# Moving a gate chain from GpSimd to VectorE, ahead of the first probabilities, with DMA reordering behind it

## Chip, cores and metric

One Trainium2 chip, one core. The metric is the device time of one execution in microseconds (us). The kernel before was timed three times: 417.96, 418.92 and 419.44 us, median 418.92. TensorE is called PE in the rows, VectorE DVE, ScalarE ACT, GpSimd POOL, and SyncE SP; "q" behind an engine's name is its instruction queue.

## The reference, cut to what matters

```python
# attention part: B=2 batches, H=8 heads, S=768 steps, D=40
for t in range(S):
    m_new  = max(f_gate[:, :, t] + m, i_gate[:, :, t])
    f_stab = exp(f_gate[:, :, t] + m - m_new)
    i_stab = exp(i_gate[:, :, t] - m_new)
    m = m_new
    C = f_stab * C + i_stab * outer(v_t, k_t)
    n = f_stab * n + i_stab * k_t
    y[:, :, t] = sigmoid(o_gate[:, :, t]) * (C @ q_t) / maximum(abs(n @ q_t), 1.0)
# mixture part: x = y as 1536 tokens x 320, E=4 experts, F=1024
p = domain_probs / (domain_probs.sum(-1) + 1e-9)
out = sum(p[:, e:e+1] * (maximum(x @ w1[e], 0) @ w2[e]) for e in range(4))
```

## The kernel before

**Tiling.** The sequence is cut into 6 chunks of 128 steps. A unit k is one chunk of one batch with its 8 heads, so there are 12 units; units 0 and 1 are the first chunks of the two batches and have nothing to carry in, units 2 to 11 are the "later units". Within a unit the recurrence is written as masked attention: scores q·k on TensorE (`first_scores`, `scores`), a decay factor per pair of steps made on ScalarE (`decays`), masked to the causal half on GpSimd (`causal`, L415), multiplied on VectorE (`probs`, L739), and taken against v on TensorE (`outputs`, L1030). `gate_x` (L757 to L769, VectorE) divides and applies the output gate, `transpose_x` (L1049 to L1051, TensorE), `xt_high` (ScalarE) and `xt_low` (VectorE) turn the result into the mixture's input.

**Gates.** The decays need, for each of 16 rows (batch, head) of the first chunks and for each of 80 rows (chunk, batch, head) of the later ones, a running maximum m and running sums. The first chunks' gate work is at the very start of VectorE's program. For the later ones, `local_maxima` scans within each chunk, `move_ends` (TensorE) brings the chunk ends to 16 rows, `unit_starts` (VectorE) scans over chunks, `move_starts` (TensorE) brings the results back to 80 rows, and `unit_maxima` (VectorE, L723 to L728) finishes m. Then GpSimd does `unit_steps` (L475 to L478), VectorE `gate_scan(1)` (L660, L665), and GpSimd `unit_sums` (L485, L486). The sums are stored to a tensor in DRAM (`g_dram`) and loaded back from it spread over 128 partitions (`load_g`, L296) or over the rows of the carried state (`load_carry`, L304), since `decays` of unit k needs them in that form. The gates' tiles are cut out of the tensor y_acc while it is free, so their rows read `y_acc`.

**Mixture.** The experts' weights come in pairs of slices (`load_pair`, 704 KB each, into `w_raw`, four pairs held at a time). Each slice w is split into a rounded high part on ScalarE (`split_high`, w_hi, L573) and a remainder (w_lo), whose 384 up columns are made on GpSimd (`split_low`, L441) and whose 320 down columns on VectorE (`split_down_low`, L776) for the first 20 slices. 128 slots M follow: in each, TensorE does `up` of a slot ahead (L1074, 8 products: high·high, low·high, high·low), ScalarE `relu`, VectorE `hidden_low` (L808), and TensorE `down(M)` (L1093). Slice w = M + 4 is split in slot M for M below 12. The work of units 2 to 11 is hung on slots: unit 2 has its first decays in slot 1, its second in slot 2, its outputs in slot 5.

**What sets the order.** Every engine's order is written out by hand, with semaphore waits; nothing is scheduled by a program. The orders around the change, before:

```python
# SP, L330-L344                              # VectorE, L831-L839
load_q(2)                                    probs(0, 0); probs(0, 1)
wait(gate_tiles[1]["ready"], 2)              unit_maxima()
store g_dram, 3 DMAs                         probs(1, 0); probs(1, 1)
load_q(3)                                    copy_keys(0, 0, U0, acc_ps[2])
wait(gate_tiles[1]["stored"], 48)            gate_x(0)
load_g(2)                                    gate_scan(1)
...                                          gate_x(1)
```

`keep_clock(n)` on TensorE multiplies a tile of ones by itself and stores nothing that is used. A tensor `*_ps` is a bank of PSUM. `d_exp` counts finished `decays`, `d_masked` finished `causal`, `p_ready` finished `probs`, `out_done` finished `outputs`.

Of the kernel before, what the change touches and what calls it, by code (L numbers as in the profile page):

```python
# [16 lines left out]
U0, U1 = B * H, NU - B * H  # L17
# [114 lines left out]
def build(nc, qk_f, qk_a, qk_s, q_p, kv_n, o_n, fi_rows, fi_units, dom_p, w_b, out):  # L132
# [4 lines left out]
    with ExitStack() as ctx:  # L137
# [143 lines left out]
        def _(sp):  # L281
# [55 lines left out]
            load_q(3)  # L337
            sp.wait_ge(gate_tiles[1]["stored"], 3 * 16)
            load_g(2)
            sp.wait_ge(out_done, 1)  # L340
            sp.wait_ge(add_done, 1)
            load_kv(sp, 2)
            load_carry(2)
            load_pair(sp, 3)  # L344
# [39 lines left out]
        def _(pool):  # L384
# [84 lines left out]
            def unit_steps():  # L469


                gt = gate_tiles[1]
                pool.wait_ge(m_ready, 1)
                pool.wait_ge(local_ready, 3)
                nc.gpsimd.tensor_tensor(gt["fm"][:, :], gt["w"][:, :], m_u[:, :], ALU.add).then_inc(unit_step, 1)  # L475
                pool.wait_ge(unit_step, 1)
                nc.gpsimd.tensor_scalar(gt["g"][:, :], gt["fm"][:, :], 0.0, None, ALU.min).then_inc(unit_step, 1)
                nc.gpsimd.tensor_scalar(gt["j"][:, :], gt["fm"][:, :], 0.0, -1.0, ALU.max, ALU.mult).then_inc(unit_step, 1)  # L478

            def unit_sums():  # L480

                gt = gate_tiles[1]
                pool.wait_ge(gt["step"], 2)
                pool.wait_ge(unit_step, 3)
                nc.gpsimd.tensor_tensor(gt["w"][:, :], gt["j"][:, :], gt["gg"][:, 0, :], ALU.subtract).then_inc(gt["ready"], 1)  # L485
                nc.gpsimd.tensor_scalar(gt["gg"][:, 1, :], gt["gg"][:, 0, :], gt["g"][:, 0:1], None, ALU.add).then_inc(gt["ready"], 1)  # L486

# [8 lines left out]
            unit_steps()  # L496
            weigh_keys(0)
            weigh_keys(1)
            unit_sums()
# [19 lines left out]
        def _(act):  # L519
# [79 lines left out]
            act.dma_start(dp[:, :, :], dom_p).then_inc(dp_in, 16)  # L599
            xt_high(0)  # L600
            xt_high(1)
            split_high(2, None)
            split_high(3, None)
# [27 lines left out]
        def _(dve):  # L631
# [98 lines left out]

            local_maxima()
            unit_starts()

# [99 lines left out]
            unit_maxima()  # L833
            probs(1, 0)
            probs(1, 1)
            copy_keys(0, 0, U0, acc_ps[2])
            gate_x(0)
            gate_scan(1)
# [73 lines left out]
        def _(pe):  # L912
# [100 lines left out]
            def outputs(k):  # L1013
# [7 lines left out]
                elif k == 1:  # L1021
                    pe.wait_ge(gate_tiles[0]["key_tok"], 1)
                elif k == B:
                    pe.wait_ge(decay_step, 3)
                else:
                    pe.wait_ge(xt_done, k)
# [79 lines left out]
            exponents_first(0, 1)  # L1106
            exponents_first(1, 0)
            exponents_first(1, 1)
            move_ends()
# [93 lines left out]
```

## Time and profile before

| | us |
|---|---|
| median of 3 runs | 418.92 |
| the profiled execution's own time | 419.46 |
| its span | 417.6 |
| TensorE busy in the span | 412.4 |
| VectorE, ScalarE, GpSimd busy | 180.2, 158.7, 152.3 |
| granted TensorE clock, mean | 0.999 |

The span begins with the first instruction recorded and ends with the last; 1.86 us of the execution's time lie around it. Busy time is the sum over instructions with overlaps counted once; a matmul's end is modelled, so that a busy TensorE may still hold small waits that show as a longer instruction.

### The profile page before, as it was taken

What the parts mean: (1) busy time and instruction counts of PE and PEld (TensorE: products, weight loads), DVE (VectorE), ACT (ScalarE), POOL (GpSimd) and SP (SyncE); (2) the same over time, 40 slices, a digit from 0 to 9 for tenths busy, and PEclk for the clock granted to TensorE, in tenths of its full rate; (3) what the DMA queues carried; (4) which work ended last, traced back from release to release, by engine and by line L of the source; (5) the groups of instructions that cost most, each with busy time, mean ns of one, the idle gap of its engine ahead of it and who ended that gap; (6) DMA issues with size and microseconds to landing.
All of it is one profiled execution on the core that took longest, in us unless ns stands there. A gap on an engine that the chain in (4) does not pass through costs nothing.

```text
span 417.6 us, 7049 instructions
## 1 busy us (share of the span) xinstructions
PE 412.4 (99%) x2710; PEld 398.7 (95%) x2710; DVE 180.2 (43%) x371; ACT 158.7 (38%) x329; POOL 152.3 (36%) x189
## 2 busy tenths in 40 slices
PE   8999999999999999999999999999999999999997
PEld 8889999999999999999999999999999999999996
DVE  5875786746554656446233231323113122131142
ACT  4575468745354644414112431143211333111111
POOL 4855835494175935304010660065100444000000
PEclk9999999999999999999999999999999999999999
DMA  7889929677513835400000232023200000010010
GB/s 268 271 261 378 390 86 346 248 267 273 187 55 104 311 129 206 129 2 1 2 2 0 75 133 71 0 71 139 71 0 2 0 0 2 0 65 0 2 63 33
DMA packets 16899, 48.45 MB, mean 116 GB/s; under 512 B 1921, under 2 KB 8594, under 8 KB 15714
## 3 DMA queue, kind: packets, MB, share of 16 engines
q1 hardware_dynamic: 16290, 46.60, 31.7%
q10 hardware_dynamic: 576, 1.40, 1.0%
q8 instruction: 22, 0.36, 0.4%
q14 instruction: 11, 0.09, 0.1%
HBM read 45.94 MB, written 2.05 MB: 115 GB/s over the span
## 4 chain that ended last, share of the span: by engine, by line
PE 94%; DMA 2%; DVE 1%; ACT 1%; POOL 1%; issue 1%; SPq 0%; DVEq 0%; POOLq 0%
PE hid_ps L1074 40%; PE acc_ps L1093 36%; PE out_ps L1030 5%; PE score_ps L1093 3%; PE out_ps L1037 2%; PE score_ps L974 2%; PE hid_ps L923 1%; PE add_ps L1009 1%; PE acc_ps L1074 1%; DMA g_all<-g_dram 1%; DMA g_dram<-y_acc 1%; PE score_ps L969 1%; ACT dec_w L552 0%; PE out_ps L1049 0%; PE out_ps L1051 0%
## 5 line engine op out<-in xcount | busy, mean ns | idle before, releaser
L808 DVE SCALAR_TENSOR_TENSOR h_lo<-hid_ps,h_hi 128x384 fp32r<-128x384 f32 (+2 forms) x120 | 68.0, 566 | 220.2 <-ACT h_hi L587 220.0
L587 ACT ACTIVATE h_hi<-hid_ps 128x384 fp32r<-128x384 f32 (+2 forms) x120 | 59.8, 498 | 233.6 <-PE hid_ps L1074 233.5
L1093 PE MATMUL acc_ps<-w_hi,h_hi 128*128 128x320 f32 x352 | 110.4, 314 | 0.1
L1093 PE MATMUL acc_ps<-w_hi,h_lo 128*128 128x320 f32 x352 | 108.8, 309 | 0.0
L1093 PE MATMUL acc_ps<-w_lo,h_hi 128*128 128x320 f32 x352 | 108.3, 308 | 0.0
L1074 PE MATMUL hid_ps<-xt_hi,w_lo 128*128 128x384 f32 (+2 forms) x360 | 103.8, 342 | 0.6 <-POOL w_lo L441 0.6
L1074 PE MATMUL hid_ps<-xt_hi,w_hi 128*128 128x384 f32 (+2 forms) x360 | 104.2, 344 | 0.1
L441 POOL TENSOR_TENSOR w_lo<-w_raw,w_hi 128x384 fp32r<-128x384 f32 x56 | 58.8, 1052 | 118.5 <-ACT w_hi L573 118.5
L1074 PEld LDWEIGHTS hid_ps<-xt_hi,w_lo 128*128 128x128 f32 x360 | 65.4, 189 | 4.9 <-POOL w_lo L441 0.8
L1093 PEld LDWEIGHTS acc_ps<-w_hi,h_hi 128*128 128x128 f32 x352 | 66.3, 188 | 1.6 <-DVE h_lo L808 0.3
L1093 PEld LDWEIGHTS acc_ps<-w_lo,h_hi 128*128 128x128 f32 x352 | 66.3, 188 | 1.3
L1093 PEld LDWEIGHTS acc_ps<-w_hi,h_lo 128*128 128x128 f32 x352 | 66.0, 188 | 0.0
L1074 PEld LDWEIGHTS hid_ps<-xt_hi,w_hi 128*128 128x128 f32 x360 | 62.4, 188 | 1.8 <-ACT w_hi L573 0.2
L1074 PE MATMUL hid_ps<-xt_lo,w_hi 128*128 128x384 f32 (+2 forms) x240 | 62.6, 342 | 0.0
L573 ACT ACTIVATE w_hi<-w_raw 128x704 fp32r<-128x704 f32 x56 | 43.6, 783 | 5.1 <-DMA w_raw<-in_w_b 5.1
L1074 PEld LDWEIGHTS hid_ps<-xt_lo,w_hi 128*128 128x128 f32 x240 | 42.7, 188 | 2.9 <-DVE xt_hi L800 0.2
L415 POOL TENSOR_SCALAR_AFFINE_SELECT dec_w<-dec_w 128x512 f32<-128x512 f32 x22 | 15.1, 685 | 60.1 <-ACT dec_w L552 60.1
L446 POOL TENSOR_TENSOR w_lo<-w_raw,w_hi 128x320 fp32r<-128x320 f32 x36 | 32.5, 902 | 0.0
L552 ACT ACTIVATE dec_w<-g_all,w_tok 128x128 f32<-128x128 f32 x80 | 25.4, 390 | 0.5 <-DMA g_all<-g_dram 0.5
L749 DVE TENSOR_TENSOR split_qk<-raw,split_qk 40x1024 fp32r<-40x1024 f32 x16 | 22.1, 1381 | 0.2
L1030 PE MATMUL out_ps<-kv,prob 128*128 128x41 f32 (+2 forms) x176 | 21.1, 280 | 0.1
L1030 PEld LDWEIGHTS out_ps<-kv,prob 128*128 128x128 f32 x176 | 20.5, 192 | 0.3 <-DVE prob L739 0.3
(171 smaller groups left out, 372.2 us busy)
## 6 DMA issues: line engine op xcount, KB each, us to landing
w_raw<-in_w_b SPq DMA_DIRECT2D x27, 704.0 KB, 4.1
raw<-in_qk_s SPq DMA_DIRECT2D x8, 1024.0 KB
g_all<-g_dram SPq DMA_DIRECT2D x10, 512.0 KB, 6.0
kv<-in_kv_n SPq DMA_DIRECT2D x12, 352.0 KB, 5.4
q_pack<-in_q_p SPq DMA_DIRECT2D x10, 192.0 KB, 6.1
out_y<-y_acc SPq DMA_DIRECT2D x12, 160.0 KB, 1.8
carry<-g_dram SPq DMA_DIRECT2D x30, 60.0 KB
y_acc<-in_o_n SPq DMA_DIRECT2D x1, 1280.0 KB, 12.3
```

Source lines behind the costliest of these rows:

```text
L415: nc.gpsimd.affine_select(out=d, in_=d, compare_op=ALU.is_ge, fill=0.0, base=0, pattern=[[0, HALF], [1, L]], channel_multiplier=-1).then_i ...
L441: up_low = nc.gpsimd.tensor_tensor(w_lo[:, f, 0:384], w_raw[:, at, 0:384], w_hi[:, f, 0:384].bitcast(fp32), ALU.subtract)
L446: nc.gpsimd.tensor_tensor(w_lo[:, f, 384:WB], w_raw[:, at, 384:WB], w_hi[:, f, 384:WB].bitcast(fp32), ALU.subtract).then_inc(w_lo_done, 1)
L552: last = nc.scalar.activation(dec(k, half)[:, a, :], e, ACT.Exp, bias=w_tok[:, k * H + h:k * H + h + 1])
L573: nc.scalar.activation(w_hi[:, f, :], w_raw[:, at, :], ACT.Copy).then_inc(w_hi_done, 1)
L587: nc.scalar.activation(h_hi[:, M % RING, 0:cols], hid_bank(M)[:, 0:cols], ACT.Relu).then_inc(hid_hi, 1)
L749: nc.vector.tensor_tensor(hi, raw[rows, kept(k), t, :, :], hi.bitcast(fp32), ALU.subtract)\
L808: nc.vector.scalar_tensor_tensor(h_lo[:, M % RING, 0:cols], hid_bank(M)[:, 0:cols], 0.0, h_hi[:, M % RING, 0:cols].bitcast(fp32), ALU.max, ...
L974: last = nc.tensor.matmul(bank[:, a * L:(a + 1) * L], split_qk[:, kept(k), 1, h, :], split_qk[:, kept(k), 0, h, :], start=True, stop=True)
L1030: last = nc.tensor.matmul(bank[:, h * DA:(h + n) * DA], prob[:, kept(k), half, at, :], values(k, h, n), start=(k < B or h == 0), stop=True ...
L1074: last = nc.tensor.matmul(hid_bank(M)[:, 0:tiles * L], w, x, start=(i == 0), stop=(i == len(terms) - 1))
L1093: last = nc.tensor.matmul(acc_ps[t][:, 0:DM], x, w, start=(f == 0 and i == 0), stop=(f == NF - 1 and i == 2))
```

## The change

- VectorE now does all gate work of the later units. `unit_maxima` and `unit_steps` come ahead of `probs(0, 0)`, `gate_scan(1)` between the probabilities of unit 0 and those of unit 1, `unit_sums` behind those of unit 1. GpSimd's program loses these five instructions.
- TensorE does `move_ends` two groups of exponents sooner and `move_starts` ahead of both `first_scores`.
- The keys' weights of the first units are turned into `hid_ps[0]` instead of `acc_ps[2]`. So `outputs(1)`, which writes `acc_ps[2]`, waits for `w_tok` only, and `keep_clock(2)` waits for `key_tok`.
- ScalarE splits slices 2 and 3 ahead of `xt_high(0)` and `xt_high(1)` instead of behind them.
- SP issues pair 3 of the weights right behind the gates' store, and `load_carry(2)` right behind `load_g(2)`.

```diff
@@ SP
-            load_q(3)
+            load_pair(sp, 3)
             sp.wait_ge(gate_tiles[1]["stored"], 3 * 16)
             load_g(2)
+            load_carry(2)
+            load_q(3)
             sp.wait_ge(out_done, 1)
             sp.wait_ge(add_done, 1)
             load_kv(sp, 2)
-            load_carry(2)
-            load_pair(sp, 3)
             load_g(3)
@@ GpSimd (the two functions are moved to VectorE, nc.gpsimd becomes nc.vector)
-            def unit_steps():
...
-            def unit_sums():
...
             causal(1, 1)
-            unit_steps()
             weigh_keys(0)
             weigh_keys(1)
-            unit_sums()
@@ ScalarE
+            split_high(2, None)
+            split_high(3, None)
             xt_high(0)
             xt_high(1)
-            split_high(2, None)
-            split_high(3, None)
@@ VectorE
+            def unit_steps():
+                gt = gate_tiles[1]
+                dve.wait_ge(m_ready, 1)
+                dve.wait_ge(local_ready, 3)
+                nc.vector.tensor_tensor(gt["fm"][:, :], gt["w"][:, :], m_u[:, :], ALU.add).then_inc(unit_step, 1)
+                dve.wait_ge(unit_step, 1)
+                nc.vector.tensor_scalar(gt["g"][:, :], gt["fm"][:, :], 0.0, None, ALU.min).then_inc(unit_step, 1)
+                nc.vector.tensor_scalar(gt["j"][:, :], gt["fm"][:, :], 0.0, -1.0, ALU.max, ALU.mult).then_inc(unit_step, 1)
+
+            def unit_sums():
+                gt = gate_tiles[1]
+                dve.wait_ge(gt["step"], 2)
+                nc.vector.tensor_tensor(gt["w"][:, :], gt["j"][:, :], gt["gg"][:, 0, :], ALU.subtract).then_inc(gt["ready"], 1)
+                nc.vector.tensor_scalar(gt["gg"][:, 1, :], gt["gg"][:, 0, :], gt["g"][:, 0:1], None, ALU.add).then_inc(gt["ready"], 1)
             local_maxima()
             unit_starts()
+            unit_maxima()
+            unit_steps()
...
             probs(0, 0)
             probs(0, 1)
-            unit_maxima()
+            gate_scan(1)
             probs(1, 0)
             probs(1, 1)
-            copy_keys(0, 0, U0, acc_ps[2])
+            unit_sums()
+            copy_keys(0, 0, U0, hid_ps[0])
             gate_x(0)
-            gate_scan(1)
             gate_x(1)
@@ TensorE, in outputs(k)
                 elif k == 1:
-                    pe.wait_ge(gate_tiles[0]["key_tok"], 1)
+                    pe.wait_ge(gate_tiles[0]["w_tok"], 1)
@@ TensorE
             exponents_first(0, 1)
+            move_ends()
             exponents_first(1, 0)
             exponents_first(1, 1)
-            move_ends()
+            move_starts()
             first_scores(0)
-            move_starts()
             first_scores(1)
             outputs(0)
             pe.wait_ge(g0["exp"], 1)
             pe.wait_ge(g0["w_tok"], 1)
-            turn(g0, "key", acc_ps[2], U0, U0, "key_ps")
+            pe.wait_ge(m_begun, 1)
+            turn(g0, "key", hid_ps[0], U0, U0, "key_ps")
             outputs(1)
             transpose_x(0)
             additions(0)
+            pe.wait_ge(g0["key_tok"], 1)
             keep_clock(2)
```

The order of VectorE's instructions from `unit_starts` to the start of `gate_x(1)`, before (line numbers of the kernel before; L739 is `probs`, L723 to L728 `unit_maxima`, L689 `copy_keys`, L757 to L769 `gate_x(0)`, L660 and L665 `gate_scan(1)`):

```order
L714 COPY y_acc<-hid_ps0 16x4
L716 SCALAR_TENSOR_TENSOR y_acc<-y_acc,hid_ps0 16x4
L739 TENSOR_TENSOR prob<-score_ps,dec_w 128x512
L739 TENSOR_TENSOR prob<-hid_ps1,dec_w 128x512
L723 TENSOR_TENSOR y_acc<-hid_ps0,y_acc 80x5
L725 TENSOR_REDUCE y_acc<-y_acc 80x1
L728 SCALAR_TENSOR_TENSOR y_acc<-y_acc 80x127
L739 TENSOR_TENSOR prob<-acc_ps0,g_all 128x512
L739 TENSOR_TENSOR prob<-acc_ps1,g_all 128x512
L689 COPY key_w<-acc_ps2 128x16
L757 TENSOR_SCALAR floor<-out_ps 128x8
```

The same stretch of VectorE in the changed kernel (its own line numbers: L702 to L707 `unit_maxima`, L716 to L719 `unit_steps`, L738 `probs`, L644 `gate_scan(1)`, L725 and L726 `unit_sums`):

```order
L702 TENSOR_TENSOR y_acc<-hid_ps0,y_acc 80x5
L704 TENSOR_REDUCE y_acc<-y_acc 80x1
L707 SCALAR_TENSOR_TENSOR y_acc<-y_acc 80x127
L716 TENSOR_TENSOR y_acc<-y_acc 80x128
L718 TENSOR_SCALAR y_acc<-y_acc 80x128
L719 TENSOR_SCALAR y_acc<-y_acc 80x128
L738 TENSOR_TENSOR prob<-score_ps,dec_w 128x512
L738 TENSOR_TENSOR prob<-hid_ps1,dec_w 128x512
L644 SCALAR_TENSOR_TENSOR y_acc<-ones,y_acc 80x127
L738 TENSOR_TENSOR prob<-acc_ps0,g_all 128x512
L725 TENSOR_TENSOR y_acc<-y_acc 80x128
L726 TENSOR_SCALAR y_acc<-y_acc 80x128
```

Six instructions of 80 rows now stand ahead of the first probabilities, a scan between the two units' probabilities, and two more ahead of the copy of the keys' weights (`copy_keys`, which follows).

SP's queue behind the gates' store (L335, L336), the difference of the two orders:

```order
 L335 DMA g_dram<-y_acc 80x128 x2
 L336 DMA g_dram<-y_acc 1x128
+L278 DMA w_raw<-in_w_b 128x1408
+L296 DMA g_all<-g_dram 128x1024
+L304 DMA carry<-g_dram 40x3x128 x3
 L310 DMA q_pack<-in_q_p 128x384
-L296 DMA g_all<-g_dram 128x1024
 L269 DMA kv<-in_kv_n 128x704
-L304 DMA carry<-g_dram 40x3x128 x3
-L278 DMA w_raw<-in_w_b 128x1408
 L296 DMA g_all<-g_dram 128x1024
```

Pair 3 moves past three loads and the wait for the store; the three loads of the carry move past one load of keys and values.

## Rows read from the trace of the kernel before

**Rows 1.** TensorE's waits in the whole span: us in total, times, longest.
```profile
PE hid_ps L1074 <- POOL w_lo L441: 0.6, 1, 0.6
PE acc_ps L1030 <- DVE key_w L689: 0.4, 1, 0.4
```

**Rows 2.** Chain that ended last, pieces: start us, us, what.
```profile
9.48 0.30 PE score_ps L987
...
11.99 1.98 PE out_ps L1030 x16
...
16.92 0.60 POOL y_acc L486
...
30.37 1.01 POOL w_lo L441
```

**Rows 3.** TensorE's timeline: start us, us, what, [idle before <- releaser].
```profile
1.15 5.49 PE L923 MATMUL hid_ps<-ones 128*128 128x128 f32 x24 [1.15 <-DVE ones L633]
...
14.49 1.95 PE L1030 MATMUL acc_ps<-kv,prob 128*128 128x123 f32 x16 [0.36 <-DVE key_w L689]
...
17.23 0.65 PE L923 MATMUL hid_ps<-ones 128*128 128x128 f32 x4
...
30.34 0.50 PE L1074 MATMUL hid_ps<-xt_hi,w_hi 128*128 128x256 f32 x2
31.43 0.50 PE L1074 MATMUL hid_ps<-xt_hi,w_lo 128*128 128x256 f32 x2 [0.59 <-POOL w_lo L441]
```

**Rows 4.** ScalarE's timeline: unit 2's decays, and splits of slices 6 and 8.
```profile
25.37 1.28 ACT L552 ACTIVATE dec_w<-g_all,w_tok 128x128 f32<-128x128 f32 x4 [0.45 <-DMA g_all<-g_dram]
...
29.49 0.79 ACT L573 ACTIVATE w_hi<-w_raw 128x704 fp32r<-128x704 f32 x1 [0.72 <-DMA w_raw<-in_w_b]
...
37.16 0.79 ACT L573 ACTIVATE w_hi<-w_raw 128x704 fp32r<-128x704 f32 x1 [4.34 <-DMA w_raw<-in_w_b]
```

**Rows 5.** SP's queue: pair 3, then pairs 4 and 5 of the weights.
```profile
23.54 0.36 SPq L278 DMA_DIRECT2D w_raw<-in_w_b  x1
...
27.40 0.84 SPq L278 DMA_DIRECT2D w_raw<-in_w_b  x2
```

**Rows 6.** Stretches: length, busy PE, PEld, DVE, ACT, POOL, then clock, DMA share, GB/s.
```profile
18.00:21.50 3.50, 3.43 (x26) 3.14 (x27) 2.89 (x6) 2.24 (x4) 3.11 (x4) 1.00 0.37 112
...
23.00:37.20 14.20, 13.61 (x99) 12.88 (x97) 8.22 (x20) 8.13 (x22) 7.30 (x9) 1.00 1.02 327
```

**Rows 7.** VectorE's timeline, 7 to 18 us.
```profile
7.63 0.26 DVE L707 TENSOR_TENSOR y_acc<-fi_u 80x128 f32<-80x128 f32 x1
...
10.65 0.69 DVE L739 TENSOR_TENSOR prob<-score_ps,dec_w 128x512 f32<-128x512 f32 x1 [0.73 <-PE hid_ps L987]
...
11.85 0.15 DVE L723 TENSOR_TENSOR y_acc<-hid_ps,y_acc 80x5 f32<-80x5 f32 x1
...
12.49 1.37 DVE L739 TENSOR_TENSOR prob<-acc_ps,g_all 128x512 f32<-128x512 f32 x2
...
17.46 0.49 DVE L769 TENSOR_TENSOR x_nat<-acc_ps,rden 128x320 f32<-128x320 f32 x1
```

**Rows 8.** GpSimd's timeline: the second and the third `causal`.
```profile
10.24 0.64 POOL L415 TENSOR_SCALAR_AFFINE_SELECT dec_w<-dec_w 128x512 f32<-128x512 f32 x1 [0.39 <-ACT dec_w L552]
...
11.27 0.64 POOL L415 TENSOR_SCALAR_AFFINE_SELECT g_all<-g_all 128x512 f32<-128x512 f32 x1 [0.34 <-ACT g_all L552]
```

**Rows 9.** VectorE's timeline: two subtractions of one shape, and the diagonal of decays.
```profile
21.56 0.85 DVE L776 TENSOR_TENSOR w_lo<-w_raw,w_hi 128x320 fp32r<-128x320 f32 x1
...
24.76 0.68 DVE L885 TENSOR_SCALAR decay_diag<-ident,decay_u 80x80 f32<-80x80 f32 x1
...
25.70 0.47 DVE L776 TENSOR_TENSOR w_lo<-w_raw,w_hi 128x320 fp32r<-128x320 f32 x1
```

**Rows 10.** GpSimd's timeline: what ran beside the first two of rows 9.
```profile
20.80 1.27 POOL L441 TENSOR_TENSOR w_lo<-w_raw,w_hi 128x384 fp32r<-128x384 f32 x1
...
24.22 1.16 POOL L441 TENSOR_TENSOR w_lo<-w_raw,w_hi 128x384 fp32r<-128x384 f32 x1 [2.16 <-ACT w_hi L573]
```

More of the change, by code:

```diff
@@ L467, in carry_state @@
                     .then_inc(state_ready, 1)
-            def unit_steps():
[L472 to L478, printed above, removed]
-            def unit_sums():
[L482 to L486, printed above, removed]
             pool.wait_ge(gate_tiles[0]["w_tok"], 1)
```

## The prediction

> **What bounds the kernel.** I read first the waits of TensorE over the whole span, since it is busy for 412.4 of 417.6 us. Beside its start and its tail it has two waits in all: 0.6 us for a weight remainder `w_lo` from GpSimd and 0.4 us for `key_w` from VectorE [rows 1]. So nothing that this change does to another engine is worth anything, except through TensorE's order before the slots run densely and through that one hole at 31 us. Then I read the chain that ended last, for what leads to the hole. It runs from the probabilities over `outputs(0)`, `gate_x`, the gate scan, GpSimd's last gate step, which ends at 16.92 + 0.60 = 17.52 us, then the store to DRAM and the load back, the decays of unit 2, and the remainder of slice 6 at 30.37 us [rows 2]. Third come the timelines. TensorE begins slot 6's `up` with two high products at 30.34 and gets to the low ones at 31.43 [rows 3]. ScalarE has its decays at 25.37 after 0.45 us of waiting for the gates from DRAM, and splits slice 6 only at 29.49, after 0.72 us of waiting for weight pair 3 [rows 4]. SP issued that pair at 23.54, behind the gates' round trip [rows 5], while from 18 to 21.5 us the DMA engines were busy for 0.37 of the time and from 23 to 37.2 us all of it [rows 6].
>
> **The hole at 31 us (SP's order, ScalarE).** Pair 3 now goes right behind the gates' store, and waits for nothing else. The store itself comes when VectorE has finished `unit_sums`, by the front part below at about 15.1 us instead of 17.52, so pair 3 is issued near 16.3, about 7 us sooner, into the thinly used stretch. Slice 6's split then isn't held by DMA: the 0.72 us go, and `w_lo` of slice 6, which needs about 1.0 us of GpSimd, ends near 30.6 at the latest instead of 31.38. It is wanted, once TensorE runs behind by the 0.6 us of the next part, at about 31.1. What the hole is worth: at least its idle 0.59 us, at most the distance between the starts, 1.09 us, less what the two high products need. Those rows overlap (0.50 us is one product's length and the other's offset), so the two need 0.2 to 0.3 us, and the wait is 0.8 to 0.9; the first of them may also have waited a little for the split. I take **0.95 us gained**. The gates from DRAM come about 2.4 us sooner, 0.45 of it would be seen by ScalarE at most, and TensorE doesn't wait there: nothing, but it keeps the hole closed.
>
> **The next weight pair.** Pairs 4 and 5 are issued at 27.40 [rows 5], and slice 8's split waits 4.34 us, to 37.16 [rows 4]. TensorE had unit 2's outputs to do meanwhile. Moved up by the 0.95 us, it would meet that wait, unless the pair lands sooner as well. It should: SP gets to it 2 to 2.4 us sooner, and one transfer of 704 KB, some 2 us at the 327 GB/s of the busy stretch [rows 6], is out of its way. Cost nothing; if DMA were not ahead by 1 us, the gain would be given back here.
>
> **The front (VectorE, TensorE, GpSimd).** This costs. Before, the first probabilities start at 10.65 [rows 7] and `outputs(0)` at 11.99 for 1.98 us [rows 2]. Now `unit_maxima` and `unit_steps` stand ahead. `move_starts` takes the place of the first scores, which began at 9.48, and takes some 0.3 us like them [rows 2], so `unit_maxima` starts near 9.85. It took 12.49 - 11.85 = 0.64 us [rows 7]. Three steps on 80 x 128 follow, at 0.26 us for the nearest row, L707 [rows 7], with their ends overlapping: 0.6 us. That makes 11.1 instead of 10.65 for the first probabilities: **0.45 us late, if nothing is in the way.** The scan of `gate_scan(1)` then lies between the probabilities; with unit 1's 1.37 us [rows 7] it fits beside `outputs(0)` as long as it takes under 1.98 - 1.37 = 0.6 us. In return `outputs(1)` no longer waits 0.36 us for `key_w` [rows 1, 3]. So the delay of `outputs(1)` is that of the first probabilities less 0.36 us. `gate_x(1)`, which ends at 17.95 [rows 7], and the start of the mixture's slots follow one for one, since only TensorE's padding at 17.23 [rows 3] lies between.
>
> **What is in the way.** The same VectorE subtraction of 128 x 320 takes 0.47 us alone and 0.85 when it starts at 21.56, during a GpSimd operation that reads SBUF until 22.07; the 80 x 80 multiplication at 24.76 takes 0.68 and ends when GpSimd's of 24.22 does [rows 9, 10]. So VectorE operations from SBUF to SBUF sat out GpSimd's. The last step of `unit_maxima` and the three `unit_steps` are of that kind, and GpSimd masks from 10.24 to 10.88 and from 11.27 to 11.91 [rows 8], just then; ScalarE sets when, and that isn't moved. Ends of the cost: no block, probabilities 0.45 late; both masks in the way, the last step done after 11.91, probabilities at about 12.15, 1.5 late. I take one mask sat out, **1.0 us late, so 1.0 - 0.36 = 0.6 us lost** behind `outputs(1)`. `unit_sums`, two steps or 0.5 us, end near 15.1 and stand ahead of `gate_x(0)`, which is hidden beside `outputs(1)` (15.1 to 17.0).
>
> The Trainium skill states it as a rule, in SBUF — State Buffer, section "Who interferes with whom": VectorE operations with two SBUF inputs, or copies and tensor_scalar in a 2-port mode, take a port pair from GpSimd exclusively, and the second to issue fully blocks. The trace agrees (0.85 against 0.47 us). Taken strictly it speaks against this change; what it would do here is rival 2.
>
> **Edits with no price.** GpSimd loses five operations and starts the remainders of slices 0 to 3 about 1 us sooner: TensorE's first `up` waits for x, not for them. Splits 2 and 3 on ScalarE now fill its idle time ahead of `xt_high(0)`; without that they would delay `relu(0)`, which isn't late. The turn into `hid_ps[0]` only enables the shorter wait. Against this, small lengthened matmuls between 20 and 39 us may shrink: 0.15 us gained.
>
> **Sum.** -0.95 - 0.15 + 0.6 = -0.5 us. The profiled execution took 419.46 us, so 418.96 for one like it; it lies 0.54 above the median of the three runs, and the difference carries over: 418.92 - 0.5 = **418.4 us**.
>
> **Rivals.**
> 1. *No block.* The front costs 0.1 us: -0.95 - 0.15 + 0.1 = -1.0, 417.9 us, with the small terms favourable 417.5. For it: a mask that comes second waits for VectorE instead, and the masks are not on the path. Against it: they are two, and 0.4 us apart.
> 2. *Every step blocked.* The last of `unit_maxima` sits out the mask until 10.88, one of the three steps that until 11.91; probabilities at 12.15, 1.5 late. The front costs 1.5 - 0.36 = 1.1 us, up to 1.5 if a pair of steps is split once more: 0.0 to +0.4, 418.9 to 419.3 us. For it: both masks lie where the steps fall. Against it: the masks leave 0.4 us between them, enough for one or two steps. The rule of the Trainium skill named above leads here.
> 3. *The hole moves.* Pair 4 doesn't land 1 us sooner, or the remainder of slice 6 is held by another thing on GpSimd: no gain, and the front's 0.6 stays: 419.5 us. For it: the DMA engines are full from 23 us on. Against: less is left to move then.
> 4. *The clock falls: slower.* TensorE is idle between the first scores, done near 12.0, and `outputs(0)`, 1.0 us or 1.5. Its first 24 products took 229 ns each, against 0.65 us for four at 17.23 [rows 3], though the granted clock reads 1.00 all along: the 1.2 GHz level, then 2.4. Should this gap bring it down, the outputs, transposes and additions up to 18 us, some 5 us of work, would take up to twice as long: +4 on top of -0.5, 422.4 us. It decides if this gap brings the level down. Against it: the stretch around 30.3 to 31.4, with 0.59 us idle and little work, left the level where it was. The Trainium skill (TensorE: Matmul & The Clock Gate, "What's actually happening") says that activity is what releases the throttle and that a lack of it brings it back; no gap in this trace shows a return.
>
> **How the numbers follow.** A measurement of this kernel can tell about 0.3%, 1.26 us, from no change: faster is below 417.66, slower above 420.18. My case 0.50 (its own range 417.9 to 418.9), no block 0.22, every step blocked 0.17, the hole moves 0.05, the clock 0.06. Of "no block" somewhat over half, and a little of my own case through unseen gains, falls below 417.66: 0.16 faster. Slower holds the clock and a small part of the others: 0.08. Same 0.76. The range leaves out the clock and the outer part of no block: 417.4 to 419.6 us.
>
> **What would show it.** The waits of TensorE without the one for `w_lo`; slot 6's high and low products 0.25 us apart; slice 6's split with no DMA wait; slice 8's split waiting less than 4.34 us. The first probabilities at 11.1 (no block), about 11.65 (mine) or past 12; a `unit_steps` operation of 0.5 us or more beside a mask shows a block. `gate_x(1)` ending near 18.5. I would be wrong if TensorE showed a new wait between 20 and 40 us, or if `outputs(0)` took more than 2.1 us (the clock).

## The result, and the profile after

The changed kernel took 422.21 us (median of 4 executions: 420.73, 422.12, 422.30, 422.32) against 418.74 for the kernel before (4 executions), a ratio of 1.0075 with a 95% interval of 1.0046 to 1.0104: 3.5 us slower, where 418.4 and a range of 417.4 to 419.6 were predicted. The profiled execution took 422.3 us with a span of 420.6.

TensorE's waits over its whole span, to set beside [rows 1]. The 0.6 us for `w_lo` and the 0.4 us for `key_w` are gone, and beside the one at the program's start there is one new wait, ahead of `outputs(0)`:

```profile
PE out_ps L1029 <- DVE prob L738: 1.5, 1, 1.5
```

TensorE's timeline of the changed kernel (start us, us, what, [idle before <- releaser]). L916 at 5.73 is the first turn of the gates, L1029 the outputs of units 0 and 1, L1092 the first product of `down(0)`, with which the dense slots begin:

```profile
1.15 4.65 PE L922 MATMUL hid_ps<-ones 128*128 128x128 f32 x24 [1.15 <-DVE ones L612]
5.73 0.23 PE L916 MATMUL acc_ps<-ident,y_acc 16*128 16x16 f32 x1
...
12.28 3.63 PE L1029 MATMUL out_ps<-kv,prob 128*128 128x123 f32 x16 [1.53 <-DVE prob L738]
...
16.06 3.64 PE L1029 MATMUL acc_ps<-kv,prob 128*128 128x123 f32 x16
...
26.49 0.31 PE L1092 MATMUL acc_ps<-w_hi,h_hi 128*128 128x320 f32 x1
```

`outputs(0)` took 1.98 us before [rows 2] and takes 3.63 now, `outputs(1)` 3.64 instead of 1.95 [rows 3]. The stretches of one microsecond say why (length, then busy PE, PEld, DVE, ACT, POOL with counts, then granted clock, DMA share, GB/s):

```profile
10.00:11.00 1.00, 0.76 (x14) 0.56 (x11) 0.96 (x4) 1.00 (x6) 0.77 (x2) 1.00 1.00 417
11.00:12.00 1.00, 0.00 (x0) 0.00 (x0) 1.00 (x3) 0.47 (x3) 0.64 (x1) 0.79 0.97 402
12.00:13.00 1.00, 0.72 (x3) 0.72 (x4) 1.00 (x4) 1.00 (x2) 0.00 (x0) 0.50 1.12 315
...
21.00:22.00 1.00, 1.00 (x7) 1.00 (x7) 0.83 (x3) 0.00 (x0) 0.73 (x1) 0.59 0.81 258
22.00:23.00 1.00, 1.00 (x11) 0.99 (x10) 0.00 (x0) 0.42 (x1) 0.00 (x0) 1.00 0.90 302
```

The granted clock goes from 1.00 (2.4 GHz) to 0.50 (1.2 GHz) at about 11.6 us, in the middle of TensorE's idle stretch, and comes back at about 21.8. The 16 products of `outputs(0)` begin at the lower level. That is rival 4 of the prediction, at its place.

VectorE's timeline shows how the first probabilities got late (L707 is the last of `unit_maxima`, L716 to L719 `unit_steps`, L738 `probs(0, 0)`, to set beside [rows 7]):

```profile
9.19 0.73 DVE L707 SCALAR_TENSOR_TENSOR y_acc<-y_acc 80x127 f32<-80x127 f32 x1
9.96 0.29 DVE L716 TENSOR_TENSOR y_acc<-y_acc 80x128 f32<-80x128 f32 x1
10.28 0.62 DVE L718 TENSOR_SCALAR y_acc<-y_acc 80x128 f32<-80x128 f32 x1
10.82 0.21 DVE L719 TENSOR_SCALAR y_acc<-y_acc 80x128 f32<-80x128 f32 x1
10.96 0.67 DVE L738 TENSOR_TENSOR prob<-score_ps,dec_w 128x512 f32<-128x512 f32 x1
```

GpSimd's second and third masks ran at 9.15 to 9.79 and at 10.19 to 10.83, and the two long operations end 0.13 and 0.07 us after them. Times in two profiles can't be compared as they stand: the 24 products of ones took 5.49 us before and 4.65 here. The granted clock reads 1.00 over both, so that the level is read from the length of the products, as in the prediction. The marks in the profile of the kernel before (the turn, the two products of `keep_clock(1)`, the first product of the exponents (`exponents_first`), and the first of `down(0)`):

```profile
6.57 0.28 PE L917 MATMUL acc_ps<-ident,y_acc 16*128 16x16 f32 x1
6.79 0.68 PE L923 MATMUL hid_ps<-ones 128*128 128x128 f32 x2
7.22 1.09 PE L931 MATMUL acc_ps<-g_parts,pick 128*128 128x128 f32 x8
...
22.50 0.31 PE L1093 MATMUL acc_ps<-w_hi,h_hi 128*128 128x320 f32 x1
```

Counted from the turn (6.57 us before, 5.73 after), the first probabilities start at 5.23 us instead of 4.08: 1.15 us late. The turn is not a clean mark, for the products of ones behind it took 0.68 us before and 0.49 in the changed kernel. Counted from the first product of the exponents (7.22 and 6.13), the first probabilities start at 4.83 instead of 3.43: 1.40 us late. The second mark leaves the slow products out and is the cleaner.

Splits of slices 6 and 8 on ScalarE, to set beside [rows 4]. Neither waits for DMA now:

```profile
32.09 0.78 ACT L552 ACTIVATE w_hi<-w_raw 128x704 fp32r<-128x704 f32 x1
...
35.71 0.78 ACT L552 ACTIVATE w_hi<-w_raw 128x704 fp32r<-128x704 f32 x1
```

**Where the time went.** Two distances separate the parts: from that turn to the first product of `down(0)` (the front), and from there to the end of the span (the slots). Before: 22.50 - 6.57 = 15.93 and 417.6 - 22.50 = 395.1. After: 26.49 - 5.73 = 20.76 and 420.6 - 26.49 = 394.1. So the slots give back 1.0 us and the front costs 4.8 us. The sum is 3.8; this execution's turn came 0.84 us sooner, which makes the 3.0 us between the spans. From the first product of the exponents, the front is 15.28 us before and 20.36 after, 5.1 us more.

### The profile page after: what moved, and what is told of

It is laid out like the page before. It is cut to its first block, busy times and chain, and to the rows that moved or that the text cites. A ratio compares the mean times of both kernels' runs of the same rounds, so it can differ in the third digit from the quotient of the medians.

```text
span 420.6 us, 7048 instructions
## 1 busy us (share of the span) xinstructions
PE 415.0 (99%) x2710; PEld 401.9 (96%) x2710; DVE 180.0 (43%) x376; ACT 158.8 (38%) x329; POOL 149.9 (36%) x184
## 4 chain that ended last, share of the span: by engine, by line
PE 97%; ACT 1%; issue 0%; DVE 0%; POOL 0%; DVEq 0%; POOLq 0%
PE hid_ps L1073 41%; PE acc_ps L1092 37%; PE out_ps L1029 5%; PE score_ps L1092 3%; PE acc_ps L1073 2%; PE out_ps L1036 2%; PE add_ps L1008 2%; PE score_ps L973 2%; PE hid_ps L922 1%; PE acc_ps L1029 1%; PE score_ps L968 1%; ACT dec_w L531 0%; PE out_ps L1048 0%; PE out_ps L1050 0%; PE out_ps L1049 0%
## 5 line engine op out<-in xcount | busy, mean ns | idle before, releaser
L1092 PE MATMUL acc_ps<-w_hi,h_hi 128*128 128x320 f32 x352 | 110.4, 314 | 0.1
L1092 PE MATMUL acc_ps<-w_hi,h_lo 128*128 128x320 f32 x352 | 108.8, 309 | 0.0
L1092 PE MATMUL acc_ps<-w_lo,h_hi 128*128 128x320 f32 x352 | 108.4, 308 | 0.0
L1092 PEld LDWEIGHTS acc_ps<-w_hi,h_hi 128*128 128x128 f32 x352 | 66.3, 188 | 1.6 <-DVE h_lo L807 0.3
L1092 PEld LDWEIGHTS acc_ps<-w_lo,h_hi 128*128 128x128 f32 x352 | 66.2, 188 | 1.3
L1092 PEld LDWEIGHTS acc_ps<-w_hi,h_lo 128*128 128x128 f32 x352 | 66.0, 188 | 0.0
L1029 PE MATMUL out_ps<-kv,prob 128*128 128x41 f32 (+2 forms) x176 | 22.8, 293 | 1.5 <-DVE prob L738 1.5
L1029 PEld LDWEIGHTS out_ps<-kv,prob 128*128 128x128 f32 x176 | 22.2, 205 | 1.7 <-DVE prob L738 1.7
```

The source lines that it names most:

```text
L1029: last = nc.tensor.matmul(bank[:, h * DA:(h + n) * DA], prob[:, kept(k), half, at, :], values(k, h, n), start=(k < B or h == 0), stop=True ...
L1092: last = nc.tensor.matmul(acc_ps[t][:, 0:DM], x, w, start=(f == 0 and i == 0), stop=(f == NF - 1 and i == 2))
```

## The experiments

Theory: TensorE idles 1.5 us ahead of `outputs(0)`, its clock falls to the lower level, and 4 us of the 4.8 are that. Rivals: the new order of VectorE and GpSimd costs by itself; the clock falls there whatever is done.

For each kernel this table gives the idle time of TensorE ahead of `outputs(0)` in its profiled execution, in how many of its executions the mean granted clock was below 0.998, the front and the slots as defined above, and the times. A front or slots with a fall in them are marked *. In the profiles of b1_pool_sums and b3_split_fill the fall comes ahead of `outputs(0)` and lengthens the first scores, so that their "none" says nothing of the executions without a fall.

| kernel | idle, us | clock fell in | front | slots | median us | ratio to before, 95% |
|---|---|---|---|---|---|---|
| before | none | 2 of 105 | 15.93 | 395.1 | 418.4 to 419.0 | |
| changed | 1.53 | 4 of 4 | 20.76* | 394.1 | 422.21 | 1.0075 (1.0046 to 1.0104) |
| e1_fill | none | 1 of 10 | 16.72 | 393.9 | 418.38 | 1.0006 (0.9984 to 1.0029) |
| e2_sp_act | none | 0 of 10 | 15.95 | 394.7 | 419.01 | 1.0005 (0.9989 to 1.0021) |
| e3_front | 1.53 | 9 of 10 | 16.66 | 394.1 | 422.19 | 1.0069 (1.0046 to 1.0092) |
| e4_gap | 1.65 | 4 of 4 | 20.37* | 394.0 | 422.70 | 1.0094 (1.0073 to 1.0115) |
| e5_hold | 1.07 | 8 of 10 | 16.26 | 394.1 | 419.56 | 1.0025 (1.0014 to 1.0036) |
| e6_gap_mid | 0.86 | 5 of 9 | 19.42* | 394.0 | 419.84 | 1.0035 (1.0020 to 1.0050) |
| b0_split | 0.53 | 0 of 11 | 15.90 | 394.1 | 417.87 | 0.9988 (0.9978 to 0.9997) |
| b1_pool_sums | none | 2 of 12 | 18.19* | 394.1 | 418.00 | 0.9995 (0.9978 to 1.0011) |
| b2_sums_fill | none | 2 of 12 | 15.69 | 397.5* | 417.70 | 0.9988 (0.9971 to 1.0006) |
| b3_split_fill | none | 3 of 12 | 18.72* | 394.1 | 418.34 | 0.9997 (0.9979 to 1.0014) |
| e7_pe_order | 0.53 | 2 of 12 | 16.06 | 395.3 | 418.99 | 1.0007 (0.9988 to 1.0026) |
| b4_dense | none | 0 of 12 | 16.47 | 394.1 | 418.63 | 0.9988 (0.9974 to 1.0001) |

The kernel before was run beside each group; its medians were 418.45 (e1 to e4), 418.42 (e5, e6, b0, b1), 418.56 (b2, b3) and 418.99 (e7, b4). Each of these four groups ran on a chip of its own. Both falls of the kernel before belong to the last group, to its 23 executions; in the other three it fell in none of 82. So counts of falls are safely compared only within a group.

From the first product of the exponents, the front is 15.28 us before, 15.29 in e2_sp_act and b2_sums_fill, 15.47 in b0_split, 15.66 in e7_pe_order, 15.80 in e5_hold, 15.91 in b4_dense, and 16.26 in both e1_fill and e3_front.

### e1_fill: the idle stretch filled

```diff
+            for _ in range(6):
+                nc.tensor.matmul(acc_ps[2][:, 384:512], ones[:, :], ones[:, :], start=True, stop=True)
             outputs(0)
```

> The changed kernel with 6 products of ones (12 passes, some 1.3 us at full rate) put between the first scores and outputs(0), in a bank that is free. Clock theory (the idle 1.53 us ahead of outputs(0) brings TensorE to 1.2 GHz): the granted clock stays 1.00 from 7 us on, outputs(0) takes 1.9 to 2.0 us instead of 3.63, and the time falls by about 4.5 to 5 us against the changed kernel, to 417.3 to 418.3. Rival theory (the later order of VectorE and GpSimd costs by itself, the clock is a bystander): the time stays within 1 us of the changed kernel's 422.2. Third (the clock falls there whatever TensorE does, as a matter of phase): the clock still reads 0.50 for about 10 us, 422.

TensorE's timeline of this kernel. L1113 is the filler:

```profile
6.57 0.28 PE L916 MATMUL acc_ps<-ident,y_acc 16*128 16x16 f32 x1
...
11.59 1.60 PE L1113 MATMUL acc_ps<-ones 128*128 128x128 f32 x12
13.18 1.98 PE L1029 MATMUL out_ps<-kv,prob 128*128 128x123 f32 x16
...
23.29 0.31 PE L1092 MATMUL acc_ps<-w_hi,h_hi 128*128 128x320 f32 x1
```

`outputs(0)` is back to 1.98 us, the clock fell in 1 of 10 executions instead of 4 of 4, and the median fell by 3.8 us, to 418.38. That is 0.1 us above the range expected, and the fall of 4.5 to 5 us that was expected came out smaller. Useless products, and nothing else, took back what the change had lost. In that profile the front is 0.79 us longer than before's from the turn, and 0.98 from the first product of the exponents. That is what the new order costs by itself.

### e4_gap and e6_gap_mid: the idle stretch put into the kernel before

```diff
+            for n in range(3):
+                wait_if(dve, pad_done, n)
+                nc.vector.memset(x_nat[:, :, :], 0.0).then_inc(pad_done, 1)
+            dve.wait_ge(pad_done, 3)
             probs(0, 0)
```

e6_gap_mid has two memsets instead of three.

> The kernel before, with three memsets in a row on VectorE ahead of the first probabilities (about 2 us, into x_nat, which is written over later) and nothing else. Clock theory: outputs(0) waits some 1.3 us, the clock falls to 0.50 for about 10 us, and the time is 1.3 us for the delay plus 4 to 5 for the clock above before: 424 to 425. Rival (a gap of that size costs itself only): 420.1.

> The kernel before with two memsets instead of three ahead of the first probabilities: outputs(0) waits about 1.0 us. Clock theory with a dose: the clock falls in fewer executions than with 1.65 us, or in none; where it stays the time is 0.8 to 1.0 us above before, 419.4, where it falls 421.5 to 422. Rival (any wait there brings it down every time): all executions near 422.

TensorE's timeline of e4_gap:

```profile
13.46 3.31 PE L1034 MATMUL out_ps<-kv,prob 128*128 128x123 f32 x16 [1.65 <-DVE prob L739]
...
26.94 0.31 PE L1097 MATMUL acc_ps<-w_hi,h_hi 128*128 128x320 f32 x1
```

Two stretches of the same profile, in the columns used above:

```profile
13.00:14.00 1.00, 0.54 (x4) 0.55 (x5) 0.93 (x5) 0.56 (x1) 0.00 (x0) 0.93 0.90 204
14.00:16.00 2.00, 2.00 (x12) 2.00 (x11) 1.24 (x3) 0.00 (x0) 1.60 (x3) 0.50 1.09 283
```

With no part of the change in it, the kernel before falls in 4 of 4 executions and takes 422.70 us. The fall was there. The time is 1.3 us below the low end expected, for two reasons that its profile shows: the level came back after about 6.8 us and not after 10, and its slots took 394.0 us instead of 395.1. The second had not been thought of. This kernel has neither the early gates nor the early pair 3, and yet TensorE no longer waits for `w_lo` of slice 6: it comes 4.4 us later, and the remainder is there. e6_gap_mid's profile shows the same, with a front 3.5 us longer. With the shorter wait, e6_gap_mid fell in 5 of 9. Its executions without a fall took 419.05, 419.25, 420.19 and 420.57 us; the two with a mean clock of 0.991 took 421.3 and 421.4. The other three, with a mean clock of 0.995 to 0.996, took 419.6 to 419.8. Within its group, on one chip, the falls go with the idle time of the profile: 0 of 11 at 0.53 us (b0_split), 5 of 9 at 0.86, 8 of 10 at 1.07 (e5_hold). In the group of e4_gap they are 9 of 10 and 4 of 4 at 1.53 and 1.65 us, and 0 and 1 of 10 in the two kernels without an idle stretch. No length parts the executions of one kernel. In e6_gap_mid's profile the fall comes at 12.5 us, when TensorE has been busy again for 0.4 us after a stretch of 0.86 (two stretches of its profile):

```profile
11.00:12.00 1.00, 0.25 (x6) 0.06 (x2) 1.00 (x3) 1.00 (x4) 0.66 (x3) 1.00 0.99 413
12.00:13.00 1.00, 0.89 (x5) 0.89 (x6) 0.93 (x5) 1.00 (x2) 0.51 (x2) 0.75 1.22 229
```

### e3_front and e2_sp_act: the change taken apart

e3_front is the changed kernel with SP's old order; e2_sp_act is the kernel before with the edits on SP and ScalarE alone.

```diff
# e3_front, SP, against the changed kernel
-            load_pair(sp, 3)
+            load_q(3)
             sp.wait_ge(gate_tiles[1]["stored"], 3 * 16)
             load_g(2)
-            load_carry(2)
-            load_q(3)
...
             load_kv(sp, 2)
+            load_carry(2)
+            load_pair(sp, 3)
             load_g(3)
```

> The changed kernel with SP's old order. Clock theory: the clock falls as in the changed kernel, and the hole at slice 6 may come back since pair 3 is issued some 3 us later: 422.2 to 423.2. If the SP order were what costs, it would be near before's 418.8.

> The kernel before with the edits on SP (pair 3, carry) and ScalarE (splits 2 and 3 sooner) alone. The hole theory (pair 3's late issue makes the wait at 31 us): slice 6's split no longer waits for DMA, the wait for w_lo goes, 0.9 us faster than before, 417.8 to 418.2. Rival (the hole depends on the gates' time, which isn't changed here): the 0.6 us wait stays and the time is before's within 0.3 us. No theory expects a fall of the clock.

e3_front's median is 422.19, so SP's order isn't what costs: as the clock theory expected. Its profiled execution is by chance the one of ten without a fall, with the same idle stretch in it:

```profile
5.48 0.23 PE L916 MATMUL acc_ps<-ident,y_acc 16*128 16x16 f32 x1
...
12.03 1.98 PE L1029 MATMUL out_ps<-kv,prob 128*128 128x123 f32 x16 [1.53 <-DVE prob L738]
...
22.14 0.31 PE L1092 MATMUL acc_ps<-w_hi,h_hi 128*128 128x320 f32 x1
```

Its front takes 16.66 us, against 20.76 in the changed kernel's profile with the same instructions on TensorE: the fall costs 4.1 us, all else 0.73 us over before (0.98 from the first product of the exponents). Its slots take 394.1 us, with pair 3 late in the queue as before.

Here the expected return of the hole did not come. Two things differ from before. With the gates' store sooner, SP gets to pair 3 at 21.68 instead of 23.54, of which 1.09 us is this execution's earlier turn; and TensorE's front is 0.73 to 0.98 us longer, so that TensorE wants the remainder of slice 6 that much later, where it used to wait 0.59 us for it. e4_gap and e6_gap_mid show that lateness alone closes the hole, there of 4.4 and 3.5 us; in e7_pe_order, with both old orders and a front 0.1 to 0.4 us longer, the wait for slice 6 is 0.2 us. So e3_front doesn't tell what the earlier gates are worth. e2_sp_act is the cleaner run, for its front is as before's. With pair 3 sooner and the gates as late as before, slice 6's split no longer waits for DMA, as expected, but TensorE still waits, for 0.25 us:

```profile
31.00 0.50 PE L1074 MATMUL hid_ps<-xt_hi,w_lo 128*128 128x256 f32 x2 [0.25 <-POOL w_lo L441]
```

Its slots take 394.7 us, so the edits on SP and ScalarE alone are worth 0.4 us of the 1.0 in the profile, which this measurement can't tell from nothing: the median is 419.01 (ratio 1.0005), and not the 417.8 to 418.2 expected. No run has the earlier gates alone at an unchanged front; the change's parts together close the hole in b0_split, below, whose front is at most 0.2 us longer than before's.

### e5_hold: the masks held until VectorE's steps are done

```diff
+            pool.wait_ge(m_ready, 1)
             causal(0, 1)
             count_weights(0)
+            pool.wait_ge(unit_step, 3)
             causal(1, 0)
```

> The changed kernel, with GpSimd's second mask held until VectorE has finished unit_maxima, and its third until unit_steps is done. Port theory (the first probabilities are late because VectorE's steps sit out GpSimd's masks): the last operation of unit_maxima falls from 0.73 to about 0.35 us and the first tensor_scalar of unit_steps from 0.62 to about 0.2, the first probabilities start 0.7 to 0.8 us sooner after the first scores, and outputs(0) waits about 0.8 us instead of 1.53. Rival (the operations are that long by themselves on 80 x 128): their durations don't change. Clock theory: with an idle stretch of about 0.8 us the clock stays up in most executions, so 417.5 to 418.5; if even that gap brings it down, 421.5.

VectorE's timeline of e5_hold (L709 is the last of `unit_maxima`, L718 to L721 `unit_steps`):

```profile
10.09 0.35 DVE L709 SCALAR_TENSOR_TENSOR y_acc<-y_acc 80x127 f32<-80x127 f32 x1
10.47 0.29 DVE L718 TENSOR_TENSOR y_acc<-y_acc 80x128 f32<-80x128 f32 x1
10.79 0.55 DVE L720 TENSOR_SCALAR y_acc<-y_acc 80x128 f32<-80x128 f32 x1
```

GpSimd's timeline, the held mask:

```profile
10.62 0.64 POOL L415 TENSOR_SCALAR_AFFINE_SELECT dec_w<-dec_w 128x512 f32<-128x512 f32 x1 [0.97 <-DVE y_acc L709]
```

The last of `unit_maxima` falls from 0.73 to 0.35 us once the mask doesn't run beside it. The first tensor_scalar stays long, because the held mask, 10.62 to 11.26, now meets that one. The two waits bought 0.47 us instead of 0.75, and the idle stretch was 1.07 us. The clock fell in 8 of 10 executions, though most of them lost less (mean clock 0.996 and 0.992, 419.3 to 420.6 us). The median, 419.56 us, is above the 417.5 to 418.5 expected for a short stretch. The port theory holds for the operation that was freed. That the second is of the same kind is seen in b1_pool_sums, where no mask runs beside the same tensor_scalar:

```profile
12.89 0.22 DVE L727 TENSOR_SCALAR y_acc<-y_acc 80x128 f32<-80x128 f32 x1
```

### Versions that might beat both

```diff
# b0_split, VectorE, against the changed kernel
             unit_maxima()
-            unit_steps()
...
             probs(0, 1)
-            gate_scan(1)
+            unit_steps()
             probs(1, 0)
             probs(1, 1)
+            gate_scan(1)
             unit_sums()
```

b1_pool_sums is b0_split with `unit_sums` on GpSimd, ahead of `weigh_keys(0)`. b2_sums_fill and b3_split_fill are b1 and b0 with two filler products ahead of `outputs(0)`. b4_dense is b2 with one product more behind `move_ends` and one behind `move_starts`. e7_pe_order is the kernel before with the change's order of `move_ends` and `move_starts` on TensorE alone.

> The changed kernel with unit_maxima still ahead of the first probabilities, but unit_steps behind those of unit 0 and the scan behind those of unit 1; SP and ScalarE as changed. By the clock theory TensorE has no idle stretch over 0.3 us ahead of outputs(0), the clock stays, the first probabilities start within 0.2 us of before's place, and the hole at slice 6 stays closed: 417.5 to 418.0, 0.7 to 1.1 us below before. Rival (what VectorE does more delays gate_x(1) as much as the hole gives back): 418.5, no change.

b0_split took 417.87 us, ratio 0.9988 (0.9978 to 0.9997), 0.5 us under before and 4.3 under the changed kernel, with no fall in 11 executions. It lies inside what was expected, but with so small a gain, in one of several versions tried, that only the interval's edge tells it from no change. Its front takes 15.90 us, as before's does (0.2 us more from the first product of the exponents), with an idle stretch of 0.53 us where under 0.3 was expected, and its slots 394.1:

```profile
12.14 1.98 PE L1029 MATMUL out_ps<-kv,prob 128*128 128x123 f32 x16 [0.53 <-DVE prob L737]
...
22.47 0.31 PE L1092 MATMUL acc_ps<-w_hi,h_hi 128*128 128x320 f32 x1
```

> As b0_split, with unit_sums back on GpSimd, ahead of its keys' weighing. VectorE is freer by 0.4 to 0.5 us ahead of gate_x(0), so the first up should start 0.2 to 0.4 us sooner than in b0_split; the store comes some 0.6 us later, which nothing waits for: 417.2 to 417.8. Rival: GpSimd's sums hold up VectorE's own operations at the shared port and nothing is gained, equal to b0_split.

Five of its 12 executions took 417.1 to 417.5, but two took 420.5 and 420.6 us, with a mean clock of 0.992, and the median, 418.00, is above the range expected. Its profiled execution is one of these, and the fall isn't where it was looked for. There is no wait of TensorE near it; it comes in the first scores, at about 9.9 us, and the granted clock reads 0.50 from 10.0 on:

```profile
9.50:9.75 0.25, 0.25 (x6) 0.23 (x7) 0.12 (x1) 0.25 (x3) 0.08 (x1) 1.00 1.18 496
9.75:10.00 0.25, 0.25 (x6) 0.25 (x6) 0.20 (x2) 0.25 (x3) 0.03 (x1) 0.77 0.93 383
```

> b1_pool_sums with two products of ones (about 0.43 us) in the idle stretch ahead of outputs(0). If that stretch is what made the clock fall in 2 of its 12 executions, none falls now and the median is 417.3 to 417.8. Rival: in b1_pool_sums's profile the clock fell near 9.9 us, ahead of that stretch, while TensorE ran small products; then the filler doesn't help, and about one execution in six is still at 420.5.

> b0_split with the same two products. It had no fall in 11 executions, so the filler has nothing to win: 417.9, within 0.2 us of b0_split; a loss of 0.1 to 0.2 us if the products end after the probabilities do.

The filler behind the first scores didn't remove this kind of fall. b3_split_fill fell in 3 of 12, on another chip, where b0_split had none, and its profile has the fall at the same place; its median is 418.34 instead of 417.9. These counts don't tell 0 of 11 from 3 of 12. Two of b2_sums_fill's 12 fell as well, though its median, 417.70, is in the range expected. Its profiled execution showed something else again, TensorE's waits being

```profile
PE acc_ps L1074 <- ACT w_hi L561: 0.7, 1, 0.7
PE acc_ps L1074 <- POOL w_lo L441: 0.6, 1, 0.6
```

and ScalarE's split of slice 8 coming only at

```profile
36.65 0.79 ACT L561 ACTIVATE w_hi<-w_raw 128x704 fp32r<-128x704 f32 x1 [6.11 <-DMA w_raw<-in_w_b]
```

That is rival 3: TensorE, 1 us ahead in that execution, ran into weight pair 4, waited 1.3 us in two pieces, and the clock was down from about 38.4 to 41.8 us. It took 420.42 us, with 397.5 us of slots instead of 394.1: 1.3 of waits, and 2.1 for the rest, the clock above all. e7_pe_order's profile has the same wait for slice 8's `w_lo`, 0.6 us, and its clock stayed up. The other executions with a full clock took 417.3 to 418.4.

> The kernel before with TensorE's new order alone: move_ends two groups of exponents sooner, move_starts ahead of both first scores; VectorE, GpSimd, ScalarE and SP as before. There is no new idle stretch on TensorE. Theory A (the falls near 9.9 us in b1_pool_sums and b3_split_fill come from this order, whose small products are spread ahead of the first scores): the clock falls in some of about 12 executions, to 421 or so, and stays in most; median 418.4 to 418.9. Theory B (those falls need what VectorE or the fillers do): no fall in any, as in all executions of the kernel before.

> b2_sums_fill with one more product of ones behind move_ends and one behind move_starts, 0.2 us each. Theory A: TensorE is denser between 8 and 10 us, the early falls go, and the median is 417.5 to 417.8 with no execution above 419. If the falls near 9.9 us come all the same, two products there are not what decides it.

e7_pe_order fell in 2 of 12 executions, to 421.5 us, for a mean clock of 0.991. On the same chip the kernel before fell in 2 of 23, to 421.0, less deep (0.995), so that theory B's "as in all executions of the kernel before" no longer holds, and 2 of 12 can't be told from 2 of 23: that TensorE's order brings the falls is not shown. "No new idle stretch" was wrong of it too: the first scores end sooner and `outputs(0)` waits 0.53 us in its profile, so its two falls may have come there; no profile shows them. b4_dense fell in 0 of 12, which doesn't settle it either. Its median is 418.63, not the 417.5 to 417.8 expected, and one execution took 420.08 with a full clock: its front is 0.5 to 0.6 us longer than before's. Beside 418.99 that is no better a ratio than b0_split's.

## Why the prediction was wrong

**The step that failed** is the clock's term. The sum has none, so that the idle stretch ahead of `outputs(0)` costs only its length; measured, the lower level that followed it costs 4.1 us more. The prediction named the mechanism, the place and the price in rival 4 (+4, 422.4 us; measured 422.21) and gave it a chance of 0.06. Some of the agreement is luck: the executions of the changed kernel lie between 420.73 and 422.32 us, with mean clocks of 0.992 to 0.988, and the gain of 0.5 us that the 4 was added to was not there in full. It gave the 0.06 on "Against it: the stretch around 30.3 to 31.4, with 0.59 us idle and little work, left the level where it was." That stretch lies in a dense run of slots and its wait is 0.59 us. The one to come was 1 to 1.5 us by the same prediction's own numbers, behind products of 40 rows. One harmless example of half the length was taken as evidence on a longer one. The runs put in its place: no idle time ahead of `outputs(0)` in the kernel before, 2 falls in 105; 0.86 us, 5 of 9; 1.07, 8 of 10; 1.5 to 1.65, 17 of 18 (the changed kernel, e3_front and e4_gap). With such a table the chance at 1.0 to 1.5 us would have been well over a half. e1_fill and e4_gap show the cause from both sides: the idle stretch filled, the loss goes; the idle stretch put into the kernel before, the loss comes.

**The hole at 31 us: right in size, open in part on its cause.** 0.95 us predicted, 395.1 - 394.1 = 1.0 measured. In the changed kernel itself this proves little, for TensorE came 4.8 us later, and e4_gap and e6_gap_mid have the same 394.0 us with none of the change. b0_split has 394.1 at a front close to before's, and there most of the gain belongs to the edits that it shares with the change. The prediction gave all of it to pair 3's place in SP's queue; e2_sp_act has that, with ScalarE's edit, and gets 0.4. What the earlier gates add was not measured by themselves. As a sum, 0.6 us lost and 0.95 gained may stand side by side, but a front that is late by more than the wait closes the hole by itself, and then the other edits have nothing left to win there. SP began the load of the gates at 19.98 us instead of 21.48, with the turn 0.84 us sooner in that profile; 2.4 us were predicted for their arrival.

**The front without the clock: right in kind, too small.** 0.6 us predicted for one mask sat out; 0.73 (e3_front) and 0.79 (e1_fill) measured from the turn, 0.98 in both from the first product of the exponents. The first probabilities were 1.15 or 1.40 us late by the two marks, instead of 1.0. Both masks were in fact met, one by the last of `unit_maxima`, one by the first tensor_scalar, as rival 2 had it, but the two cost 0.38 and 0.40 us (0.73 instead of 0.35, 0.62 instead of 0.22), less than a mask's 0.64 each. So the price fell between my case and rival 2's 1.1. The rule of the Trainium skill (SBUF — State Buffer, "Who interferes with whom"), that the second operation to issue fully blocks, agrees in kind, and e5_hold shows it on the first. In size it is looser than that: the last of `unit_maxima` ends 0.13 us after the mask, and not its own 0.35. That `outputs(1)`'s delay is the probabilities' delay less 0.36 us held: `outputs(0)` starts 1.13 us later from the turn and 1.38 from the exponents, and less 0.36 that is 0.77 and 1.02, beside fronts 0.73 to 0.79 and 0.98 us longer.

**The small terms** (0.15 us gained) can't be told from the rest. The slots' 1.0 us holds them and the hole together.

**The next weight pair.** Hidden in the changed kernel, where TensorE came 4 us later. It landed sooner, as predicted: slice 8's split waits 2.5 us in e1_fill and b0_split instead of 4.34, and TensorE doesn't wait for it. In e7_pe_order TensorE waited 0.6 us for it, and in b2_sums_fill, where TensorE was earliest, the rival's price was near: about 1.3 us of wait, and a short fall of the clock on top that had not been thought of.

**Without the fall** the sum would have been 0.75 - 1.0 = -0.25 us by the turn, and 0.0 by the exponents: no change that could be measured. Half the predicted gain or more was not there either.

## What to carry to other kernels

Work put ahead of the first result that TensorE waits for is priced in two parts: the delay, and what the idle stretch does to TensorE's clock afterwards. Here the second, 4.1 us, was more than four times the first, and a filler of 1.6 us of useless products took it back. Look at the granted clock of several executions, not at one profile: e3_front's profiled execution was the one in ten that looked fine. When a chain has to start sooner, put each piece where TensorE still has work: the same steps between the two units' probabilities (b0_split) cost the front 0.2 us at most and kept the whole gain of the slots. And price a gain further down together with a delay ahead of it: in e4_gap the delay alone closed the same hole.

## What the hardware showed that was not expected

- The level fell with waits as short as 0.86 us (5 of 9 executions), and in two profiles with none near it (b1_pool_sums, b3_split_fill), at about 9.9 us among the first scores, which follow products of two and five columns. With 0.86 and 1.65 us (e6_gap_mid, e4_gap) it fell only when TensorE had been busy again for 0.4 us, with 1.53 us (the changed kernel) it fell in the middle of the wait. The same instructions with the same wait fell in one execution and not in another.
- Once down, the level stayed down for about 10.2 us in the changed kernel's profile and about 6.8 in those of e4_gap, e6_gap_mid, b1_pool_sums and b3_split_fill, though TensorE was busy for nearly all of it. The Trainium skill (TensorE: Matmul & The Clock Gate, "What's actually happening") says that activity releases the throttle; the runs show that it did so only after that long.
- Two waits, 1.3 us together, at 37 to 38.6 us, in the middle of the slots, brought the level down as well, within the second of them, from about 38.4 to 41.8 us (b2_sums_fill). The second by itself, of 0.6 us, did not in e7_pe_order.
